# Clustered attention and two MLPs: guard tiles and similarities of the first four heads in another order, and a lead of two pairs

## What is computed

```python
q_assign = argmax(einsum('bhsd,hcd->bhsc', q_n, c_n))   # the same for k
mask = q_assign[:, :, :, None] == k_assign[:, :, None, :]
scores = where(mask, scale * q @ k.T, -1e9)
attn = exp(scores - max(scores)) / sum                  # then attn @ v
h = x @ w_in;  g = max(h, 0) + alpha * min(h, 0);  y = g @ w_out
h2 = y @ w_in2;  g2 = P(h2) / Q(h2);  out = g2 @ w_out2
```

## Time and profile before

| what | value |
|---|---|
| median of 3 runs | 812.85 us (812.04 to 813.98) |
| the profiled execution, its own time | 812.46 us |
| its span in the trace | 810.7 us |
| PE busy | 787.2 us, 97% of the span |
| DVE, ACT, POOL busy | 555.3, 488.2, 295.6 us |
| attention | about 0 to 261 us |

### The profile page before, as it was taken

The page is one execution under the profiler, slowest core; times in us unless marked ns, Lnnn a source line. Parts: engine busy times, 40 slices in busy tenths (PEclk is TensorE's granted clock), DMA queues, the critical chain, the costliest instruction groups (busy, mean ns, idle before and its releaser), DMA issues.

```text
span 810.7 us, 13124 instructions
## 1 busy us (share of the span) xinstructions
PE 787.2 (97%) x4344; PEld 745.2 (92%) x4344; DVE 555.3 (68%) x949; ACT 488.2 (60%) x838; POOL 295.6 (36%) x330
## 2 busy tenths in 40 slices
PE   6897999999999999999999999999999999999997
PEld 5787899999998999999999999998998899988896
DVE  5656787787775555543454445468888888888886
ACT  3754777777778311211121134378999999999996
POOL 7864779888975599000000017540000000000000
PEclk9998999999999999999999999999999999999999
DMA  7622754753640323000000015420001001001001
GB/s 198 181 75 75 184 132 108 199 130 103 168 112 23 121 83 113 15 0 0 0 0 0 0 52 156 122 61 1 1 1 39 0 0 39 0 0 39 1 1 39
DMA packets 30311, 52.15 MB, mean 64 GB/s; under 512 B 9182, under 2 KB 11323, under 8 KB 30267
## 3 DMA queue, kind: packets, MB, share of 16 engines
q1 hardware_dynamic: 30266, 51.59, 23.1%
HBM read 29.40 MB, written 3.19 MB: 40 GB/s over the span
## 4 chain that ended last, share of the span: by engine, by line
PE 82%; DVE 9%; ACT 6%; issue 2%; POOL 1%; DMA 1%; SPq 0%; ACTq 0%; DVEq 0%; POOLq 0%
PE ps L207 28%; PE ps L1196 16%; PE ps L1207 12%; PE ps L727 4%; PE ps L760 4%; PE ps L773 4%; PE ps L812 4%; PE ps L804 4%; PE ps L805 4%; PE ps L698 2%; DVE g_f L1358 1%; ACT scratch L1274 1%; DVE corr L1345 1%; ACT scratch L1272 1%; DVE g_f L1348 1%
## 5 line engine op out<-in xcount | busy, mean ns | idle before, releaser
L213 ACT ACTIVATE g_hi<-g_f 128x384 fp32r<-128x384 f32 x128 | 67.4, 526 | 216.9 <-PE ps L1196 193.5
L217 DVE TENSOR_TENSOR g_lo<-g_f,g_hi 128x384 fp32r<-128x384 f32 x128 | 79.2, 619 | 81.7 <-ACT g_hi L213 81.7
L207 PE MATMUL ps<-x_hi,w_hi_b 128*128 (+1 forms) x352 | 118.8, 337 | 0.0
L207 PE MATMUL ps<-x_hi,w_lo_b 128*128 (+1 forms) x352 | 118.7, 337 | 0.0
L207 PE MATMUL ps<-x_lo,w_hi_b 128*128 (+1 forms) x352 | 118.7, 337 | 0.0
L940 ACT ACTIVATE probs_hi<-ps 128x768 fp32r<-128x768 f32 x96 | 78.1, 814 | 64.1 <-PE ps L773 63.3
L1054 DVE TENSOR_REDUCE row_max<-ps 128x1 fp32r<-128x768 f32 x96 | 90.9, 949 | 36.6 <-PE ps L727 36.5
L390 DVE TENSOR_TENSOR probs_lo<-ps,probs_hi 128x768 fp32r<-128x768 f32 x64 | 60.9, 952 | 20.1 <-ACT ps L943 20.0
L390 POOL TENSOR_TENSOR probs_lo<-probs,probs_hi 128x768 fp32r<-128x768 f32 x32 | 59.2, 1850 | 33.2 <-ACT probs L943 33.2
L225 DVE TENSOR_SCALAR corr<-ps,alpha_c 128x384 f32<-128x384 f32 x64 | 39.5, 617 | 46.3 <-PE ps L207 46.1
L1377 POOL TENSOR_TENSOR w_lo_a<-stage,w_hi_a 128x512 fp32r<-128x512 f32 x10 | 13.3, 1361 | 157.1 <-ACT w_hi_a L1294 157.1
(11 more groups left out here) (132 smaller groups left out, 2088.6 us busy)
## 6 DMA issues: line engine op xcount, KB each, us to landing
stage<-in_moe_w_in SPq DMA_DIRECT2D x27, 256.0 KB, 2.6
stage<-in_moe_w_out SPq DMA_DIRECT2D x27, 256.0 KB, 2.8
raw<-in_qk SPq DMA_DIRECT2D x16, 384.0 KB, 3.7
op_a<-head_hi SPq DMA_DIRECT2D x32, 192.0 KB, 3.2
v_raw<-in_v SPq DMA_DIRECT2D x16, 192.0 KB, 2.5
op_b<-head_hi SPq DMA_DIRECT2D x16, 192.0 KB, 3.4
op_b<-head_lo SPq DMA_DIRECT2D x16, 192.0 KB, 3.2
scratch<-spread SPq DMA_DIRECT2D x16, 192.0 KB, 4.5
```

Source lines behind the costliest of these rows:

```text
L207: last = pe.matmul(h_ps[j % H_RING][:, 0:BLK], a[:, 0, w], x[:, kt, cols], start=(kt == 0 and i == 0), stop=(kt == KT - 1 and i == 2))
L213: act.activation(g_hi[:, j % 2], g_f[:, j % 2], ACT.Copy).then_inc(g_hi_made, 1)
L217: dve.tensor_tensor(g_lo[:, j % 2], g_f[:, j % 2], g_hi[:, j % 2].bitcast(F32), ALU.subtract)\
```

## The change

- The order of the list for heads 0 and 1 is new on PE, DVE and POOL. `turn_onehot(1)` stands before `weigh_hi(0)`, and DVE makes that onehot before the guard tile (0,4). `sim(3)` stands in pair 4 and `sim(4)` in pair 8, in front of guard (2,1). The second guard tile of a pair with two moves to another pair.
- The similarity of head 3 goes to bank 7 too, behind that of head 2 in the same bank (`SIM_AT`).
- `turn_onehot(4)`, `put_mask_q(4)` and `put_mask_k(4)` move from s = 1 to s = 0 of head 2, like those of the other heads.
- Head 4 is halved too (`HALVED = 5`): one `turn_max`, one `take_max` and one `put_max` more.
- From head 4 on the guard tile of a pair is the one two pairs ahead (`AHEAD = 2`) instead of three, and `turn_max` of the next head stands at s = 4 instead of s = 3. `put_max` follows it.
- On POOL `mark_nearest(3)` goes ahead of `make_lo(6)`, `split_w(0)` goes behind it, and `split_head(4)` is no longer cut in two.

The core of the diff:

```diff
-            SIM_BANK = {1: 7, 2: 7}
+            SIM_AT = {1: (7, 0), 2: (7, 0), 3: (7, T * 2 * C)}
...
-            HALVED = 4
+            HALVED = 5
...
-            GUARD = {(2, 0): {2: (3, 0)}, (2, 1): {2: (3, 1)}, (2, 2): {3: (3, 2)}, (2, 3): {2: (3, 3), 3: (3, 4)},
...
-            TURNED = {(2, 0): (2, 1), (2, 3): (3, 0), (2, 5): (3, 1), (3, 4): (4, None)}
+            AHEAD = 2
+            GUARD = {(2, 0): {1: (2, 5), 3: (3, 0)}, (2, 1): {2: (3, 1)}, (2, 2): {3: (3, 2)}, (2, 3): {2: (3, 3)},
+                     (2, 4): {1: (3, 4), 3: (3, 5)}, (2, 5): {2: (4, 0)}, (3, 0): {2: (4, 1)}, (3, 1): {2: (4, 2)},
+                     (3, 2): {2: (4, 3)}, (3, 3): {1: (4, 4), 3: (4, 5)}, (3, 4): {2: (5, 0)}, (3, 5): {2: (5, 1)}}
+
+            TURNED = {(2, 3): (3, 0), (2, 5): (3, 1), (3, 2): (4, 0), (3, 4): (4, 1)}
...
-                regular = {3 if s == 2 else 2: (n + 1, s + TH) if s < TH else (n + 2, s - TH)}
+                t = s + AHEAD
+                regular = {3 if s == 2 else 2: (n + 1, t) if t < T else (n + 2, t - T)}
...
-                return (n + 1, None) if s == 3 and n + 1 < N else None
+                return (n + 1, None) if s == T - AHEAD and n + 1 < N else None
...
-                return {3: T * 2 + 2, 4: T * 2 + 4, 5: T * 3 + 1, 6: T * 4 + 3}.get(m, T * (m - 1) - 2)
+                return {4: T * 2 + 1, 5: T * 3 + 1, 6: T * 4 + 2}.get(m, T * (m - 2) + AHEAD + 1)
...
-            BEHIND_SIM = {(2, 2): 3, (2, 4): 4, (3, 2): 5, (4, 4): 6}
-
-            def turn_pair(n):
-
-                return 1 if n == 2 else 0
+            BEHIND_SIM = {(2, 2): 4, (3, 2): 5, (4, 3): 6}
...
-                        if s == turn_pair(n) and n + 2 < N:
+                        if s == 0 and n + 2 < N:
                             turn_onehot(n + 2)
...
+                    if g == WRITTEN_OUT * U:
+                        turn_max(2, 1)
...
-                        pe.wait_ge(sim_taken, 4 if (m, h) == (2, 0) else min(m + 3, N))
+                        pe.wait_ge(sim_taken, 5 if m == 2 else min(m + 3, N))
```

More of the change, by code:

```diff
@@ L517, in _ @@
                         put_max(3, 1)
+                    elif n == 3:
+                        put_max(4, 0)
+                        put_max(4, 1)
                     elif n + 1 < N:
@@ L843, in _ @@
                 score(1)
+                turn_onehot(1)
                 weigh_hi(0)
@@ L846, in _ @@
                 score(2)
-                turn_onehot(1)
+                weigh_hi(1)
                 turn_max(0, 1)
-                weigh_hi(1)
                 weigh_lo(0)
+                guard(1, 0)
+                sim(2)
                 score_a(3)
                 weigh_lo(1)
-                guard(1, 0)
-                sim(2)
                 guard(1, 1)
@@ L858, in _ @@
                 weigh_hi(2)
+                sim(3)
+                score(4)
                 guard(1, 2)
-                score(4)
                 weigh_lo(2)
+                weigh_hi(3)
                 turn_max(1, 0)
                 guard(1, 3)
-                weigh_hi(3)
                 score(5)
                 weigh_lo(3)
+                weigh_hi(4)
                 guard(1, 4)
-                weigh_hi(4)
                 turn_onehot(2)
+                weigh_lo(4)
                 score(6)
-                weigh_lo(4)
                 guard(1, 5)
@@ L880, in _ @@
                 guard(2, 0)
-                guard(2, 1)
                 weigh_hi(6)
                 score(8)
-                sim(3)
+                sim(4)
+                guard(2, 1)
                 weigh_lo(6)
                 weigh_hi(7)
+                score(9)
                 guard(2, 2)
-                score(9)
+                turn_onehot(3)
                 weigh_lo(7)
+                weigh_hi(8)
+                score(10)
                 turn_max(2, 0)
                 guard(2, 3)
-                weigh_hi(8)
-                turn_onehot(3)
-                score(10)
-                sim(4)
                 weigh_lo(8)
                 weigh_hi(9)
+                score(11)
                 guard(2, 4)
-                score(11)
                 weigh_lo(9)
-                guard(2, 5)
                 for g in range(WRITTEN_OUT * U, UNITS + LAG):
@@ L1098, in _ @@
                 first_nearest(2)
+                nearest(3)
                 take_guard(1, 2)
@@ L1103, in _ @@
                 take_guard(1, 4)
+                ranked(3)
                 take_guard(1, 5)
+                first_nearest(3)
                 take_max(1, 1)
@@ L1108, in _ @@
                 take_guard(2, 1)
-                nearest(3)
+                nearest(4)
                 make_lo(dve, U + 2)
                 take_guard(2, 2)
-                ranked(3)
-                first_nearest(3)
+                ranked(4)
+                first_nearest(4)
                 take_max(2, 0)
                 take_guard(2, 3)
-                nearest(4)
                 make_lo(dve, U + 4)
-                ranked(4)
-                first_nearest(4)
                 take_guard(2, 4)
                 make_lo(dve, U + 5)
-                take_guard(2, 5)
                 for g in range(WRITTEN_OUT * U, UNITS):
```

41 lines of the change are left out of this document (18 added, 23 removed).

## The result

The changed kernel took **802.09 us** (median of 4 runs, 801.23 to 803.20) against 812.72 us before (812.04 to 813.98): ratio 0.9868, 95% interval 0.985 to 0.9886, 10.6 us by the medians. The forecast was 802.2 us, so the size and the sign were right. Run a second time, beside 11 runs of before, it gave 801.89 us against 812.44 us, ratio 0.9874 (0.9854 to 0.9895).

The account below looks back on a forecast made before the run. PE's work bounds the kernel; only its losses in heads 0 to 3 can be won. 14.3 us lost, less 3.7 of remaining waits and 0.1 for the added turn_max, gains 10.5 us: forecast 802.2 us, range 799.3 to 807.6.

Parts of the forecast that it names:

- The loss of before: Heads 0 to 3: PE loses 14.3 us there (10.4 waits, 1.3 behind them, 2.6 clock); from head 4 nothing to win.
- Onehot of head 1: DVE, head 1: from_first takes 0.36 us instead of 2.03, onehot ready about 20.4 us, PE waits 0.3 instead of 1.3.
- The mask and the clock: Before weigh_hi(12): the 2.54 us wait for head 4's mask goes, with 2.6 us lost to 5.3 us at half clock.
- The other waits left: Heads 0 to 3 after the change: 2.7 us of waits in 9 places, the longest 0.8 us at the maximum (2,1).
- 0.11 us behind each wait: Two matmuls behind each PE wait take 0.62 us instead of 0.51: 1.3 us for 12 waits.
- The lead of two at nothing: From head 4 on: one guard tile (0.35 us) less before head 4, one more in pair (14,3), set against itself.
- The maximum in later heads: Later heads: put_max issued 3.4 us before its score, landing at the median 2.2 us; no wait, 1.2 us slack.
- The rival's mechanism: Heads 5 to 15: put_max's DMA takes 4.6 us, first scores wait 1.2 us each, 815.2 us; chance 0.03.
- The rival of a DVE that takes PE's place: Heads 2 and 3: DVE's full queue (15.1 against 15.3 us) brings waits back, 807.0 us; chance 0.17.
- SP and POOL at nothing: load_w(3) on SP waits for POOL's split_w(1) ahead of put_max(2,1); done some 6 us early, costed at nothing.

Follow-up runs that it names:

- the two experiments: Mask of head 4 written first in pair 13 in the kernel before: 807.26 us; changed kernel with that mask late again: 807.54 us.
- the single guard tile: Kernel before with only guard (2,1) moved behind score(8) and sim(3) on PE: 811.72 us, ratio 1.0002.
- the lead alone: Kernel before with guard tiles two pairs ahead and the maximum at s = 4 from head 4, one tile less in head 3: 810.96 us, ratio 0.9979.
- the lead of three: Changed kernel with AHEAD = 3, tile (5,2) added in pair (3,5) and the maximum at s = 3 from head 4: 804.55 us, ratio 0.9903.
- The three parts together: Kernel before with the early mask of head 4, the early onehot of head 1 and the lead of two pairs: 805.49 us, ratio 0.9922.
- the mask alone: Kernel before with one edit, DVE writing the mask of head 4 first in pair 13: 807.26 us, ratio 0.9933.
- the kernel with the late maximum: Changed kernel with SP issuing put_max of later heads only after the first exponential of the last pair: 823.84 us, ratio 1.0134.

## Why the prediction was right, point by point

**The loss of before.** All of it in heads 0 to 3: held. 11.0 of the 11.3 us of the profiled spans lie before head 4, and in the second profiled execution, whose span is 10.9 us shorter than that of before, 11.0 again.

**Onehot of head 1.** I said ready at 20.4 and a wait of 0.3 us; it was ready at 20.01, and PE came at 20.32 without waiting. `from_first` 0.36 us as said. What I had not seen is how the two orders hang together: with PE's new order the old place on DVE costs 5 us, with the old order 0.5 to 1.3, not settled.

**The mask and the clock.** 2.54 us of wait and 2.6 us of clock made 5.1 us; the two experiments gave 4.5 to 5.4 and 5.5. The mask ended at 56.05 us, 1.2 us before `weigh_hi(12)`. But 2.6 is the value of one execution (there the lower level lasted from 64.59 to 70.27 us, 5.7 us, so it lost 2.8). The mean clock of 50 executions of before lay between 0.995 and 1.000, in half of them at 0.998; an execution with 0.998 (that of the single guard tile) shows 2.8 us of work at the lower level, half of which is lost. By the mean clock 0.998 is 1.6 us. So 1.4 to 1.6 us is the commoner price, and this mis-sized term is 1 us too large for the medians.

**The other waits left.** 2.7 us in nine places said, 1.7 in five listed. But the list is not all: a matmul of 384 columns is shown with 0.34 us while the next one could start after 0.17, so each listed wait is 0.17 us longer than listed, and waits of up to 0.28 us are found in the starts that the list does not have. In the changed kernel, PE and DVE:

```profile
63.86 0.51 PE L807 MATMUL ps<-probs_lo,v_hi 128*128 128x384 f32 x2
64.38 0.62 PE L722 MATMUL ps<-op_a 128*128 128x384 f32 x2
```

```profile
63.36 0.96 DVE L1042 TENSOR_REDUCE row_max<-ps 128x1 fp32r<-128x768 f32 x1 [0.15 <-PE ps L722]
```

Two such pairs start 0.35 us apart in an unbroken sequence, these 0.52; the second is guard (3,5), and the reduction it needs ended at 64.32 us. Guards (4,1) and (4,5), at 69.29 and 79.03 us, start late by 0.16 and 0.21 us, 0.05 us behind the end of a reduction too. Measured by such starts, what I had counted was there in eight of nine places (late by, and in brackets what I said): the maximum (2,1) 0.53 (0.8), guards (3,4) and (4,4) 0.43 and 0.43 (0.35, 0.45), guards (1,0), (2,2), (4,1), (4,5) 0.23, 0.21, 0.16, 0.21 (0.2, 0.1, 0.1, 0.3) and the maximum (4,0) 0.20 (0.1); only onehot(1) came without a wait (0.3). That is 2.4 us for my 2.7. Not foreseen were 0.48 at `sim(4)`, 0.60 at guard (5,1) behind the long `ranked`, now the longest (I had named the maximum), and 0.5 us in sum at three more places. So the waits left are 4.0 us and not 2.7; by the same measure those of before are 13.0 us and not 10.4.

**0.11 us behind each wait.** This is the step that failed. The price itself was right: the two matmuls behind each of the listed waits on a guard tile start 0.28 us apart instead of 0.17. But I took it for all that a wait costs beside its listed length, 1.3 us for twelve, and took the list for all waits. The 0.17 us that each listed wait is longer make 2.0 us for the twelve and 0.85 for the five, 1.2 us for the change. The short waits that no list shows stand against it: eight in the changed kernel, 1.5 us, and three before, 0.6 us. They are most of what the starts of matmuls with no listed wait between them, from 22.3 us to head 4, lie further apart in sum than 0.172 us each: 3.2 us before (5.8, less the 2.6 of the clock), and 4.1 us in the changed kernel. By these starts the gain up to head 4 would be 13.0 - 4.0 + 2.6 + 0.35 for the tile not done - 0.1, 11.85 us, and 11.0 were measured; the 0.8 us between them were not found at one place.

**The lead of two at nothing.** The tile set against itself: before head 4 it is saved; what it costs in pair (14,3) can't be seen, since from head 13 on the two profiled executions of the changed kernel lie 0.7 us below and 0.2 us above that of before. The 1.7 us of the lead alone are no extra term: the lead took away the wait of 0.98 us at the end of head 3, which my 10.4 us held already, and a tile; what is left is less than half the width of the interval.

**The maximum in later heads.** No wait, as said; the issue came 3.65 us before its score instead of 3.4 (3.54 in most heads, 2.8 and 2.9 in the last two, which I had not told apart), and the landing is 1.95 us, not 2.2. The rival's mechanism is real: delayed to behind the exponentials, the same transfer makes the kernel slower than before. Its length is not: at 4.6 us, which I took from another kind of row transfer, nothing was seen; those transfers landed in 2.0 to 5.3 us in the changed kernel, and the maximum's never was late there. The rival of a DVE that takes PE's place showed in small, 1.0 us of listed waits in heads 2 and 3, and 1.8 us in the lead of three.

**SP and POOL at nothing.** No wait of PE for either from 20 to 90 us but the 0.32 at `sim(4)`, put down to issue, which means that the profile shows nothing it waited for; its cause stays open.

So the forecast was right by its mechanism: the waits named went, the mask's with its clock, and those foreseen stayed. It was right to a tenth by luck. The waits removed were 9.0 us and not 7.7, 1.3 us too little in my sum; the clock was 1 us too much for the medians, and 0.8 us of loss was not in it at all.

**What stays open.** The three parts together gain 7.2 us. The remaining 3.4 us are what the rest of the change gives: the order of similarities, guards and onehots of heads 0 to 3, the halved head 4, the bank of `sim(3)` and POOL's order. By the waits of 1.34, 0.62 and 0.95 us that go with it they belong to the new order, but this is argued from the trace; none of these parts was run by itself.

## What to carry to other kernels

A wait at the head of a queue is removed by moving the one instruction it waits for past those that nobody wants yet, as with the mask; in a list of small waits for the same engine a tile moved alone may only bring the engine sooner to the next thing that isn't ready (1.34 us here became 0.76 us one tile later), so move producer and consumer together. Before a reordering is called free, ask which instruction it makes more urgent, and measure that one late. A list of waits is not the whole of what an engine loses: compare the starts of instructions with those of an unbroken sequence before you put prices on it. And look at a second profiled execution before you explain a difference of half a microsecond.

## What the runs showed of the hardware that was not expected

The same 2.54 us wait was followed by 5.3 us and more at the 1.2 GHz level in one execution, and by about 3 us in those of three other kernels (2.8, 3.2 and 3.3 us); one of before's runs had a mean clock of 1.000 and took 810.34 us, three with 0.999 took 809.5 to 810.8, five with 0.995 took 813.8 to 814.0. Without that wait the changed kernel's eight executions all had 0.999 or 1.000, and lie within 2 us. A wait of 1.34 us was not followed by the lower level in the profiled execution of before, one of 1.63 us was in the kernel with the late maximum.

The slow pairs of the start (0.84 us for two matmuls) ended at 19 to 20.5 us in most executions and at 22.1 us in two. The profile shows a granted clock of 1.00 there in all of them, but the starts speak for the lower level: such pairs start 0.64 us apart (19.51 and 20.15 in the mask alone), and so do those in the stretch of before that has 0.50 in its row:

```profile
66.00 0.84 PE L760 MATMUL ps<-op_a 128*128 128x384 f32 x2
66.64 0.84 PE L773 MATMUL ps<-op_b 128*128 128x384 f32 x2
```

Elsewhere they start 0.35 us apart. So when the start ended, and with it what the onehot of head 1 was worth, looks like a matter of the clock that the profile's column does not show.
